# Order and buffers at the seam between attention and the gated layer of a fused fp32 kernel

## The chip, the cores and the metric

The kernel runs on one core of a Trainium2 chip. The metric is the device time of one execution in microseconds (us), median over the runs. The engines are named as in the profile: PE is TensorE (matmuls; PEld its weight loads), DVE is VectorE, ACT is ScalarE, POOL is GpSimd, SP is SyncE, whose queue issues the DMAs. The engines run side by side, each its own instructions in order, and meet through semaphores.

## The reference

Three stages follow each other, all in fp32. B = 4 batches, 8 heads, 1152 tokens that are pooled in twos to 576 queries, head size 64.

```python
def _attn_ref(q, k, v):
    q_pool = q.reshape(B, H, S // 2, 2, D).mean(axis=3)
    scores = (1 / sqrt(D)) * q_pool @ k.transpose(0, 1, 3, 2)
    attn = softmax(scores)                      # with 1e-9 in the sum
    return attn @ v                             # x: (4, 576, 512)

def _moe_ref(x, w_in, g_ln, w_sg, b_sg, w_out):
    h = gelu(x @ w_in)                          # tanh form, (4, 576, 1024)
    u, v = h[..., :512], h[..., 512:]
    v_n = (v - mean(v)) / sqrt(var(v) + 1e-6) * g_ln
    v_s = einsum('ts,bsd->btd', w_sg, v_n) + b_sg[None, :, None]
    return x + (u * v_s) @ w_out
```

A third stage (a token and a channel product with residuals) follows and isn't touched.

## The kernel before

**Attention.** The 32 heads go in 16 pairs (NP = 16; i is the pair). A pair has NS = 9 steps: steps 0 to 3 are query tiles of head 0, step 4 the remainder of both heads, steps 5 to 8 tiles of head 1. A step's work is a pipeline over the engines: PE makes the scores (L687, or L673 to L675 for step 4), DVE takes them out of PSUM with the row maximum (`take`, L1140), ACT makes the exponentials (`exps`, L950), DVE the reciprocal of the sum (`recip`, L1147 and L1149), POOL the normalisation (`norm`, L541), PE 18 transposes of it (`transpose_p`, L638), ACT and DVE copy these out to the tile pT (`evac_p`, L937 and L1155). The transposes of a step are made LAG = 4 steps after its scores. The value products of a pair (`values`, L704) are spread over the steps of the next pair by PV_STEPS: steps 0 to 3 hold head 0, steps 4 to 8 head 1. A finished head is copied from its PSUM bank to the tile xT by ACT and DVE together (`acc_copy`, L937 and L1160; semaphores acc_by_act and acc_by_dve).

After the last pair the same nine steps run once more without scores (`tail=True`, i = NP, L741, L983, L1184): this is the drain. Its steps 0 to 3 still transpose and evacuate steps 5 to 8 of the last pair, and hold the values of head 0; steps 4 to 8 hold only the values of head 1.

**Gated layer.** Products are made in fp32 out of three products of rounded parts: each operand is split in a high part (fp32r, a copy) and a low part (the difference). x of a batch is four slabs of 128 channels by 576 tokens: ACT copies to x_h (`x_hi_of`), DVE subtracts to x_l (`x_lo_of`, L1197). w_sg is split likewise in five rows (`sg_hi` on ACT, `sg_lo` on DVE, L1202). The weights are split by POOL (L501 the copy, L549 the subtraction), two units of them for w_out (wo) at the start of this layer.
PE makes in the order of the list GELU the value tiles v0 and v1 (`v_tile(b, m)`, 12 matmuls of 512 columns), then u0 (`pair(b, 0)`, 24 matmuls of 288), v2, v3, v4, u1, u2, u3. Each of them goes through the gelu: ACT `square`, DVE `poly` (L1209), ACT `tanh`, DVE `gelu` (L1226 for v, to the tile v_f). A v tile is then normalised: DVE statistics (L1229, L1230, L1232 to var_e), POOL the power (`norm_rstd`, L600), DVE `norm_v` (L1239), ACT n_h, DVE `norm_lo` (L1247). v_tile(b, 2) waits until gelu(b, 0) has freed its PSUM bank, v_tile(b, 3) for gelu(b, 1). DVE's order in batch 0 is gelu(0, 0), poly(0, 2), norm_v(0, 0), gelu(0, 1).

**The seam.** The tiles of the gated layer (context ctx2) lie over those of attention (ctx1) in the order in which both are declared. PE (L831, L832), ACT (L987), DVE (L1188), POOL (L591) and SP (L469) all wait there for acc_by_act and acc_by_dve to reach 2 * NP, that is, for the last copy of the last head. Then ACT copies the four x_h slabs, sg_hi(0), sg_hi(1), square(0, 0) and so on, DVE subtracts the x_l slabs, and PE starts v_tile(0, 0), which waits for x_split slab by slab. POOL starts its split of wo, and SP loads b_row, g_col and the weights of the third stage.

Of the kernel before, what the change touches and what calls it, by code (L numbers as in the profile page):

```python
# [27 lines left out]
PV_STEPS = ((0, range(0, 3)), (0, range(3, 5)), (0, range(5, 7)), (0, range(7, 9)),  # L28
            (1, range(0, 1)), (1, range(1, 3)), (1, range(3, 5)), (1, range(5, 7)), (1, range(7, 9)))
# [6 lines left out]
def at(i, per, off):  # L36

    return i * per + off
# [16 lines left out]
def build(nc, q, k, v, x_w_in, g_ln, w_sg, b_sg, w_out, w_tok1, w_tok2, w_ch1, w_ch2, out):  # L55
    NP, _, S = k.shape
    B, D = out.shape[0], v.shape[-1]
    H = 2 * NP // B
    SQ = S // 2
    DM = H * D  # L60
    KT_N = DM // P
    FF = x_w_in.shape[1]
    HF = FF // 2
# [4 lines left out]
    SPP = NP // B  # L68
# [3 lines left out]
    TT = QT_N  # L72
# [8 lines left out]
    def rows(t):  # L81
        return P if t < TT - 1 else QL
# [19 lines left out]
    def sb(ctx, name, shape, dt=F32):  # L102
        return ctx.enter_context(nc.sbuf_tensor(name, shape, dt))

    def sem(name):
        return top.enter_context(nc.semaphore(name))

    with top:
        ps = top.enter_context(nc.psum_tensor("ps", [P, 8, 512], F32))
        ident = sb(top, "ident", [P, P])  # L110
        xT = sb(top, "xT", [P, NP, SQ])
# [8 lines left out]
        ctx1 = ExitStack()  # L120
# [6 lines left out]
        ql2 = sb(ctx1, "ql2", [P, 2, QC], F32R)  # L127
        k_over = sb(ctx1, "k_over", [P, 2, 2, CK], F32R)
        q_over = sb(ctx1, "q_over", [P, 2, 4 * P], F32R)
        v_sb = sb(ctx1, "v_sb", [P, 2, KB, D])  # L130
        prob = sb(ctx1, "prob", [P, P_BUFS, S])
        ctx0 = ExitStack()
        k_two = sb(ctx0, "k_two", [P, S])
        q_two = sb(ctx0, "q_two", [P, 2, 4 * P])
# [10 lines left out]
        rsum = sb(ctx1, "rsum", [P, NS])  # L145
        ctx1.close()

        ctx2 = ExitStack()
        sg_h = sb(ctx2, "sg_h", [P, TT, SQ], F32R)
        sg_l = sb(ctx2, "sg_l", [P, TT, SQ], F32R)  # L150
        wo_h = sb(ctx2, "wo_h", [P, HF // P, DM], F32R)
        wo_l = sb(ctx2, "wo_l", [P, HF // P, DM], F32R)
        b_row = sb(ctx2, "b_row", [P, SQ])
        g_col = sb(ctx2, "g_col", [P, HF // P])
        x_h = sb(ctx2, "x_h", [P, KT_N, SQ], F32R)
        x_l = sb(ctx2, "x_l", [P, KT_N, SQ], F32R)
        n_h = sb(ctx2, "n_h", [P, TT, HF], F32R)
        n_l = sb(ctx2, "n_l", [P, TT - 1, HF], F32R)
        u_T = sb(ctx2, "u_T", [P, HF // P, SQ])
        gbuf = sb(ctx2, "gbuf", [P, 3, SQ])  # L160
        v_f = sb(ctx2, "v_f", [P, 3, HF])
        bst = sb(ctx2, "bst", [P, 3, 6])
        mv = sb(ctx2, "mv", [P, 3, 2])
        var_e = sb(ctx2, "var_e", [P, 3])
        rstd = sb(ctx2, "rstd", [P, 3])
        mixed = sb(ctx2, "mixed", [P, SQ])
        gate = sb(ctx2, "gate", [P, 2, SQ])
        ctx2b = ExitStack()
        sb(ctx2b, "behind_attention", [P, SG_PAD])
        sg_raw = sb(ctx2b, "sg_raw", [P, TT, SQ])  # L170
# [58 lines left out]
        s_taken = sem("s_taken")  # L229
# [8 lines left out]
        acc_by_act = sem("acc_by_act")  # L238
        acc_by_dve = sem("acc_by_dve")
# [3 lines left out]
        x_hi = sem("x_hi")  # L243
        x_split = sem("x_split")
# [372 lines left out]
        def _(pe):  # L617
# [120 lines left out]
                    step(i + 1, 0, s)  # L738
            for s in range(NS):
                step(NP - 1, 1, s)  # L740
            for s in range(NS):  # L741
                step(NP, 0, s, tail=True)

            def three(acc, wh, wl, xh, xl, start, stop):
# [14 lines left out]
            def v_tile(b, m):  # L759

                r = rows(m)
                if m == 4:
                    pe.wait_ge(res_done, at(b, 4, RES_N - 1))
                else:
                    pe.wait_ge(gelu_done, at(b, GT, GELU_N + (V_AT[m - 2] + 1 if m >= 2 else 0)))
                if m == 0 and not isinstance(b, int):
                    pe.wait_ge(mix_done, at(b, 4, -3))
                acc = ps[0:r, V_BANK[m], :]
                for kt in range(KT_N):
                    sl = slice(m * P, m * P + r)  # L770
                    if m == 0:
                        pe.wait_ge(x_split, at(b, KT_N, kt + 1))
                    ins = three(acc, x_h[:, kt, sl], x_l[:, kt, sl], wi_h[:, kt, HF:FF], wi_l[:, kt, HF:FF],
                                kt == 0, kt == KT_N - 1)
                ins.then_inc(v_mm, 1)
# [52 lines left out]
                    pair(b, 8 + f, [(wo_h[:, kt, sl], wo_l[:, kt, sl], g_h[:, kt, :], g_l[:, kt, :])  # L828
                                    for kt in range(HF // P)])

            pe.wait_ge(acc_by_act, 2 * NP)  # L831
            pe.wait_ge(acc_by_dve, 2 * NP)  # L832
            pe.wait_ge(w_split, U_WO)
            v_tile(0, 0)
            v_tile(0, 1)
            with pe.Fori(0, B - 1) as b:
                gated(b, False)
            gated(B - 1, True)
# [94 lines left out]
        def _(act):  # L933
            sc = nc.scalar

            def copy(o, i_):
                return sc.activation(o, i_, ACT.Copy)  # L937
# [27 lines left out]
            def step(i, s, first=False, tail=False):  # L965

                if s >= LAG and not tail:
                    evac_p(i, s - LAG)
                elif s < LAG and not first:
                    evac_p(i - 1, s - LAG + NS)  # L970
                if not first and s in (TAIL_STEP - 1, NS - 1):
                    acc_copy(i - 1, 0 if s == TAIL_STEP - 1 else 1)
                if s >= 1 and not tail:
                    exps(i, s - 1)
                elif s == 0 and not first:
                    exps(i - 1, NS - 1)
# [3 lines left out]
            with act.Fori(1, NP) as i:  # L980
                for s in range(NS):
                    step(i, s)
            for s in range(NS):  # L983
                step(NP, s, tail=True)


            act.wait_ge(acc_by_act, 2 * NP)  # L987
            act.wait_ge(acc_by_dve, 2 * NP)

            def slab(b):  # L990
                return xT[:, bass.ds(b * SPP, SPP), :]

            def x_hi_of(b):
                for f in range(KT_N):
                    copy(x_h[:, f, :], xT[:, b * SPP + f, :]).then_inc(x_hi, 1)

            def sg_hi(j):
                copy(sg_h[:, j, :], sg_raw[:, j, :]).then_inc(sgT_hi, 1)

            def square(b, e):  # L1000
                kind, n = GELU[e]
                if kind == "v":
                    act.wait_ge(v_mm, at(b, TT, n + 1))
                else:
                    act.wait_ge(pair_mm, at(b, 12, n + 1))
                act.wait_ge(gelu_done, at(b, GT, e + 1))
                h, buf = gelu_of(e)

                sc.activation(buf, h, ACT.Square, scale=(0.044715 * GC) ** 0.5).then_inc(squared, 1)
# [25 lines left out]
                    square(b + 1, 1)  # L1035
                    tanh(b + 1, 0)

            x_hi_of(0)
            act.wait_ge(sg_in, 32)
            sg_hi(0)  # L1040
            sg_hi(1)
            square(0, 0)
            sg_hi(2)
            square(0, 1)
            sg_hi(3)
            sg_hi(4)
            tanh(0, 0)
# [55 lines left out]
        def _(dve):  # L1103
            ve = nc.vector
# [52 lines left out]
            def acc_copy(i, a):  # L1157

                dve.wait_ge(acc_ready, at(i, 4, 2 * a + 2))
                ve.tensor_copy(xT[PH * a:PH * a + PH, i, HALF:SQ], ps[PH:P, ACC_BANK, 0:HALF]).then_inc(acc_by_dve, 1)  # L1160

            def step(i, s, first=False, tail=False):

                if s >= LAG and not tail:
                    evac_p(i, s - LAG)
                elif s < LAG and not first:
                    evac_p(i - 1, s - LAG + NS)
                if s >= 2 and not tail:
                    recip(i, s - 2)
                elif s < 2 and not first:  # L1170
                    recip(i - 1, s - 2 + NS)
                if not first and s in (TAIL_STEP - 1, NS - 1):
                    acc_copy(i - 1, 0 if s == TAIL_STEP - 1 else 1)
                if not tail:
                    take(i, s)
                    if first:
                        first_q(s)
# [3 lines left out]
            with dve.Fori(1, NP) as i:  # L1181
                for s in range(NS):
                    step(i, s)
            for s in range(NS):  # L1184
                step(NP, s, tail=True)


            dve.wait_ge(acc_by_act, 2 * NP)  # L1188
            dve.wait_ge(acc_by_dve, 2 * NP)

            def slab(b, f):
                return xT[:, b * SPP + f, :]

            def x_lo_of(b):
                for f in range(KT_N):
                    dve.wait_ge(x_hi, at(b, KT_N, f + 1))
                    ve.tensor_tensor(x_l[:, f, :], slab(b, f), x_h[:, f, :].bitcast(F32), ALU.subtract)\  # L1197
                        .then_inc(x_split, 1)

            def sg_lo(j):  # L1200
                dve.wait_ge(sgT_hi, j + 1)
                ve.tensor_tensor(sg_l[:, j, :], sg_raw[:, j, :], sg_h[:, j, :].bitcast(F32), ALU.subtract)\  # L1202
                    .then_inc(sgT_lo, 1)

            def poly(b, e):

                dve.wait_ge(squared, at(b, GT, e + 1))
                h, buf = gelu_of(e)
                ve.scalar_tensor_tensor(out=buf, in0=buf, scalar=GC, in1=h, op0=ALU.add, op1=ALU.mult)\  # L1209
                    .then_inc(z_ready, 1)  # L1210
# [86 lines left out]
                    ve.tensor_tensor(x_f, ps[:, b0:b0 + 2, 0:HALF], x_f, ALU.add).then_inc(res_done, 1)  # L1297

            head = Chain(dve, gelu_chain, 0)
            x_lo_of(0)  # L1300
            sg_lo(0)
            sg_lo(1)
            poly(0, 0)
            sg_lo(2)
            poly(0, 1)
            sg_lo(3)
            sg_lo(4)
            gelu(0, 0, head)
# [103 lines left out]
```

## Time and profile before

| | us |
|---|---|
| median of 3 runs | 1042.06 |
| lowest and highest run | 1040.93, 1042.2 |
| the profiled execution | 1043.86 |
| its span, first to last instruction | 1042.0 |
| busy in it: PE | 1004.9 |
| DVE | 590.4 |
| ACT | 452.6 |
| POOL | 381.7 |
| mean granted clock of PE, share of full | 0.988 |

All positions in the text are us from the start of the span. Busy shares are averages over stages with different limits; what one stage waits for is read from the timeline of that stage. Matmuls overlap in the pipeline, so a group's length is a little under the sum of its means. A page row and a row of a timeline merge neighbouring instructions of a kind: "8.09 ... x4" means four instructions in 8.09 us. The granted clock in a list of windows is 1.00 at 2.4 GHz and 0.50 at 1.2 GHz.

### The profile page before, as it was taken

Reading aid. Unit: us, or ns where it says so; the run is one execution under the profiler, and the core shown is the slowest. Engines: PE = TensorE matmul, PEld = TensorE weight load, DVE = VectorE, ACT = ScalarE, POOL = GpSimd, SP = SyncE. Lnnn points to the kernel's source line nnn. Section 1 sums busy time; section 2 is a strip of 40 time slices with the busy share of each in tenths; the row PEclk is TensorE's granted clock in tenths of the full one; section 3 lists DMA queues with packets and bytes.
Section 4 is the critical chain, followed back from the end, with each engine's and each line's share of the span. In section 5 each row is a group of like instructions: output and inputs, shape, how many; then the busy total and the mean of one; then the engine's idle time right before and its main releaser. Section 6 shows DMA issues by size and latency. Waiting matters only on the chain.

```text
span 1042.0 us, 23588 instructions
## 1 busy us (share of the span) xinstructions
PE 1004.9 (96%) x8948; PEld 824.1 (79%) x8948; DVE 590.4 (57%) x1167; ACT 452.6 (43%) x851; POOL 381.7 (37%) x296
## 2 busy tenths in 40 slices
PE   7899999999999998979999999999999999999998
PEld 7677777777777766659999998988888888888898
DVE  5787878777777776669495857445312113121121
ACT  3677777777777776635151514143111101111011
POOL 3877777777777786531010102278000000000000
PEclk9899999999999999989999999999999999999999
DMA  5644444444444433310000000133000101001010
GB/s 163 191 115 114 113 113 113 113 113 113 113 113 113 113 88 95 122 37 1 1 0 0 0 0 2 53 104 108 1 1 1 40 0 40 0 0 40 0 41 21
DMA packets 34017, 65.40 MB, mean 63 GB/s; under 512 B 6208, under 2 KB 14784, under 8 KB 33984
## 3 DMA queue, kind: packets, MB, share of 16 engines
q1 hardware_dynamic: 33824, 64.34, 21.6%
q10 hardware_dynamic: 160, 0.59, 0.2%
q8 instruction: 24, 0.39, 0.2%
q14 instruction: 9, 0.07, 0.0%
HBM read 42.93 MB, written 4.72 MB: 46 GB/s over the span
## 4 chain that ended last, share of the span: by engine, by line
PE 68%; issue 22%; DVE 5%; POOL 2%; DMA 1%; ACT 0%; DVEq 0%; SPq 0%; POOLq 0%; ACTq 0%
PE ps L704 13%; PE ps L746 12%; PE ps L747 12%; PE ps L748 12%; PE ps L687 10%; PE ps L638 6%; DVE prob L1140 2%; PE ps L673 1%; POOL rstd L600 1%; DVE pT L1155 1%; PE ps L675 1%; PE ps L674 1%; DMA q_two<-in_q 1%; DMA q_raw<-in_q 0%; POOL prob L541 0%
## 5 line engine op out<-in xcount | busy, mean ns | idle before, releaser
L1140 DVE TENSOR_SCALAR_CACHE_REDUCE prob<-ps 128x1152 f32<-128x1152 f32 x144 | 195.5, 1358 | 73.9 <-PE ps L687 55.4
L541 POOL TENSOR_SCALAR prob<-prob,rsum 128x1152 f32<-128x1152 f32 x144 | 176.8, 1228 | 115.8 <-DVE rsum L1149 115.4
L950 ACT ACTIVATE prob<-prob,nmax 128x1152 f32<-128x1152 f32 x144 | 181.1, 1258 | 17.1 <-DVE prob L1140 10.3
L704 PE MATMUL ps<-pT,v_sb 128*64 128x288 f32 x1152 | 173.1, 423 | 2.5 <-DVE xT L1160 0.6
L1360 DVE SCALAR_TENSOR_TENSOR f_l<-ps,f_h 128x512 fp32r<-128x512 f32 (+1 forms) x60 | 38.3, 638 | 222.7 <-ACT f_h L1090 222.7
L937 ACT ACTIVATE pT<-ps 128x512 f32<-128x512 f32 (+1 forms) x288 | 109.5, 432 | 100.0 <-PE ps L638 99.9
L1090 ACT ACTIVATE f_h<-ps 128x512 fp32r<-128x512 f32 (+1 forms) x60 | 33.3, 555 | 256.4 <-PE ps L748 256.4
L687 PE MATMUL ps<-k_over,q_over 64*128 64x288 f32 x744 | 132.7, 311 | 4.0 <-DVE prob L1140 4.0
L687 PEld LDWEIGHTS ps<-k_over,q_over 64*128 64x128 f32 x744 | 103.7, 187 | 24.2 <-DVE prob L1140 22.7
L638 PEld LDWEIGHTS ps<-ident,prob 64*128 64x128 f32 x2592 | 100.3, 140 | 20.8 <-issue 20.7
L638 PE MATMUL ps<-ident,prob 64*128 64x64 f32 x2592 | 107.7, 225 | 6.6 <-POOL prob L541 3.6
L704 PEld LDWEIGHTS ps<-pT,v_sb 128*64 128x64 f32 x1152 | 72.1, 137 | 44.8 <-issue 9.0
L1155 DVE COPY pT<-ps 128x512 f32<-128x512 f32 x144 | 98.9, 687 | 12.7 <-PE ps L638 12.7
L747 PE MATMUL ps<-u_l,c_h 128*128 128x512 f32 (+1 forms) x240 | 88.3, 368 | 0.0
L746 PE MATMUL ps<-u_h,c_h 128*128 128x512 f32 (+1 forms) x240 | 88.3, 368 | 0.0
L748 PE MATMUL ps<-u_h,c_l 128*128 128x512 f32 (+1 forms) x240 | 88.3, 368 | 0.0
L746 PE MATMUL ps<-f_h,c_h 128*128 128x512 f32 (+1 forms) x240 | 88.3, 368 | 0.0
L747 PE MATMUL ps<-f_l,c_h 128*128 128x512 f32 (+1 forms) x240 | 88.3, 368 | 0.0
L748 PE MATMUL ps<-f_h,c_l 128*128 128x512 f32 (+1 forms) x240 | 88.3, 368 | 0.0
L687 PE MATMUL ps<-kh,qh 64*128 64x288 f32 x248 | 85.9, 346 | 0.0
L600 POOL TENSOR_TENSOR rstd<-var_e,minus_half 128x1 f32<-128x1 f32 (+1 forms) x20 | 15.5, 775 | 174.9 <-DVE var_e L1232 174.9
L687 PE MATMUL ps<-kl,qh 64*128 64x288 f32 x248 | 72.9, 294 | 0.0
(141 smaller groups left out, 2175.6 us busy)
## 6 DMA issues: line engine op xcount, KB each, us to landing
q_raw<-in_q SPq DMA_DIRECT2D x16, 640.0 KB, 5.0
k_raw<-in_k SPq DMA_DIRECT2D x16, 576.0 KB, 4.0
v_sb<-in_v SPq DMA_DIRECT2D x32, 288.0 KB, 2.8
k_over<-kh SPq DMA_DIRECT2D x31, 144.0 KB, 2.5
k_over<-kl SPq DMA_DIRECT2D x31, 144.0 KB, 2.6
out_x<-xT SPq DMA_DIRECT2D x4, 1024.0 KB, 4.2
q_over<-qh SPq DMA_DIRECT2D x31, 128.0 KB, 2.3
q_over<-ql SPq DMA_DIRECT2D x31, 128.0 KB, 2.4
```

The costliest lines, as they stand in the source:

```text
L541: g.tensor_scalar(sl, sl, rsum[:, s:s + 1], 0.0, ALU.mult, ALU.add).then_inc(norm_done, 1)
L638: ins = te.transpose(dst, prob[half, PROB_BUF[s], j * P:(j + 1) * P], ident[half, half])
L687: ins = te.matmul(ps[:, 2 * m + t, 0:CK], w, x, start=(term == 0), stop=(term == 2))
L704: ins = te.matmul(ps[PH * c:PH * c + PH, ACC_BANK, 0:n], v_sb[:, a, j, :], pT[:, a, j, c * n:c * n + n], start=(j == 0), stop=(j == KB - 1))
L746: te.matmul(acc, wh, xh, start=start, stop=False)
L747: te.matmul(acc, wh, xl, start=False, stop=False)
L748: return te.matmul(acc, wl, xh, start=False, stop=stop)
L937: return sc.activation(o, i_, ACT.Copy)
L950: sc.activation(sl, sl, ACT.Exp, scale=-1.0, bias=nmax[:, s:s + 1], accum_out=esum[:, s:s + 1]).then_inc(exp_done, 1)
L1140: ve.tensor_scalar(prob[:, PROB_BUF[s], :].rearrange("p (c n) -> p c n", c=SCORE_BANKS), ps[:, 0:SCORE_BANKS, 0:CK], -SCALE, BIG, ALU.mult ...
L1155: ve.tensor_copy(pT_of(s, 1), trans(1)).then_inc(pT_by_dve, 1)
L1360: ve.scalar_tensor_tensor(out=f_l[:, f % F_N, 0:n], in0=ps[:, f % F_N, 0:n], scalar=0.0, in1=f_h[:, f % F_N, 0:n].bitcast(F32), op0=ALU.ma ...
```

## The change

The tiles of ctx2 are declared in another order: x_h, x_l, sg_h, sg_l first, which puts them where k, q and their splits were; then gbuf, v_f, the small ones, n_h, gate, mixed; wo_h, wo_l, n_l, u_T, b_row, g_col come last of them. In ctx1, prob and v_sb exchange places. The waits of PE, ACT and DVE for the last copy of the accumulator are gone at this place; those of POOL and SP stay. ACT and DVE run only steps 0 to 3 of the drain, with the splits of x of batch 0 between them, and copy head 1's result later, behind square(0, 1) on ACT and behind poly(0, 1) on DVE. PE runs steps 0 to 3 of the drain, then v_tile(0, 0) and v_tile(0, 1), then the values of head 1.

```diff
-        v_sb = sb(ctx1, "v_sb", [P, 2, KB, D])
         prob = sb(ctx1, "prob", [P, P_BUFS, S])
+        v_sb = sb(ctx1, "v_sb", [P, 2, KB, D])
...
         ctx2 = ExitStack()
+        x_h = sb(ctx2, "x_h", [P, KT_N, SQ], F32R)
+        x_l = sb(ctx2, "x_l", [P, KT_N, SQ], F32R)
         sg_h = sb(ctx2, "sg_h", [P, TT, SQ], F32R)
         sg_l = sb(ctx2, "sg_l", [P, TT, SQ], F32R)
...
             for s in range(NS):
                 step(NP - 1, 1, s)
-            for s in range(NS):
+            for s in range(TAIL_STEP):
                 step(NP, 0, s, tail=True)
...
-            pe.wait_ge(acc_by_act, 2 * NP)
-            pe.wait_ge(acc_by_dve, 2 * NP)
+            pe.wait_ge(s_taken, NP * NS)
             pe.wait_ge(w_split, U_WO)
             v_tile(0, 0)
             v_tile(0, 1)
+            for s in range(TAIL_STEP, NS):
+                values(NP - 1, *PV_STEPS[s])
...
-            act.wait_ge(acc_by_act, 2 * NP)
-            act.wait_ge(acc_by_dve, 2 * NP)
...
-            x_hi_of(0)
+            step(NP, 0, tail=True)
+            x_hi_tile(0, 0)
+            step(NP, 1, tail=True)
+            x_hi_tile(0, 1)
+            step(NP, 2, tail=True)
+            x_hi_tile(0, 2)
+            x_hi_tile(0, 3)
+            step(NP, 3, tail=True)
             act.wait_ge(sg_in, 32)
             sg_hi(0)
             sg_hi(1)
             square(0, 0)
             sg_hi(2)
             square(0, 1)
+            acc_copy(NP - 1, 1)
             sg_hi(3)
             sg_hi(4)
             tanh(0, 0)
...
-            dve.wait_ge(acc_by_act, 2 * NP)
-            dve.wait_ge(acc_by_dve, 2 * NP)
...
-            x_lo_of(0)
+            step(NP, 0, tail=True)
+            step(NP, 1, tail=True)
+            x_lo_tile(0, 0)
+            step(NP, 2, tail=True)
+            x_lo_tile(0, 1)
+            x_lo_tile(0, 2)
+            step(NP, 3, tail=True)
+            x_lo_tile(0, 3)
             sg_lo(0)
             sg_lo(1)
             poly(0, 0)
             sg_lo(2)
             poly(0, 1)
+            acc_copy(NP - 1, 1)
             sg_lo(3)
             sg_lo(4)
             gelu(0, 0, head)
```

`x_hi_tile(b, f)` and `x_lo_tile(b, f)` are the bodies of the loops of `x_hi_of` and `x_lo_of`, one slab each.

## Rows read from the trace of the kernel before

**Rows 1.** The page, part 1: busy time, share of the span, instructions.
```profile
PE 1004.9 (96%) x8948; PEld 824.1 (79%) x8948; DVE 590.4 (57%) x1167; ACT 452.6 (43%) x851; POOL 381.7 (37%) x296
```

**Rows 2.** Windows, PE: window, length, PE busy, granted clock, DMA share, GB/s.
```profile
411.20:413.50 2.30, 0.21 (x4) 1.00 0.04 16
413.50:420.30 6.80, 5.87 (x56) 0.50 0.16 47
...
451.04:461.20 10.16, 7.24 (x16) 0.50 0.23 66
```

**Rows 3.** Timeline, PE: start, length, line, operation, count, [idle before <-releaser].
```profile
438.49 0.77 PE L638 MATMUL ps<-ident,prob 64*128 64x64 f32 x18
...
442.97 4.59 PE L704 MATMUL ps<-pT,v_sb 128*64 128x288 f32 x36 [0.64 <-DVE xT L1160]
450.01 0.47 PE L746 MATMUL ps<-wi_h,x_h 128*128 128x512 f32 x1 [2.45 <-DVE x_l L1197]
...
452.76 0.79 PE L746 MATMUL ps<-wi_h,x_h 128*128 128x512 f32 x1 [1.83 <-DVE x_l L1197]
...
462.58 0.30 PE L746 MATMUL ps<-x_h,wi_h 128*128 128x288 f32 x1
...
466.09 0.50 PE L746 MATMUL ps<-wi_h,x_h 128*128 128x512 f32 x1
...
469.09 0.50 PE L746 MATMUL ps<-wi_h,x_h 128*128 128x512 f32 x1
```

**Rows 4.** Timeline, DVE, at the seam and in the first gelus of batch 0.
```profile
438.27 0.16 DVE L1149 RECIPROCAL rsum<-lsum 128x1 f32<-128x1 f32 x1
...
447.60 0.46 DVE L1160 COPY xT<-ps 64x288 f32<-64x288 f32 x1 [4.73 <-PE ps L704]
448.97 8.09 DVE L1197 TENSOR_TENSOR x_l<-xT,x_h 128x576 fp32r<-128x576 f32 x4 [0.91 <-ACT x_h L937]
...
448.97 0.89 DVE L1197 TENSOR_TENSOR x_l<-xT,x_h 128x576 fp32r<-128x576 f32 x1 [0.91 <-ACT x_h L937]
...
452.63 4.43 DVE L1197 TENSOR_TENSOR x_l<-xT,x_h 128x576 fp32r<-128x576 f32 x2
...
467.89 0.54 DVE L1239 TENSOR_SCALAR v_f<-v_f,mv,rstd 128x512 f32<-128x512 f32 x1
468.35 0.68 DVE L1226 SCALAR_TENSOR_TENSOR v_f<-gbuf,ps 128x512 f32<-128x512 f32 x1
```

**Rows 5.** Timeline, POOL: the last normalisation, the first split of wo, the first rstd.
```profile
438.60 1.23 POOL L541 TENSOR_SCALAR prob<-prob,rsum 128x1152 f32<-128x1152 f32 x1 [0.54 <-DVE rsum L1149]
448.21 1.04 POOL L501 TENSOR_SCALAR wo_h<-stage 128x1024 fp32r<-128x1024 f32 x1 [8.39 <-DVE xT L1160]
449.34 2.75 POOL L549 TENSOR_TENSOR wo_l<-stage,wo_h 128x1024 fp32r<-128x1024 f32 x1
...
467.25 0.56 POOL L600 TENSOR_TENSOR rstd<-var_e,minus_half 128x1 f32<-128x1 f32 x1 [10.80 <-DVE var_e L1232]
```

**Rows 6.** Groups up to 520 us: line, engine, operation, count, busy, mean ns, idle before.
```profile
L549 POOL TENSOR_TENSOR wi_l<-stage,wi_h 128x1024 fp32r<-128x1024 f32 x4 | 9.5, 2379 | 0.0
...
L1202 DVE TENSOR_TENSOR sg_l<-sg_raw,sg_h 128x576 fp32r<-128x576 f32 x5 | 3.6, 749 | 0.0
```

**Rows 7.** Timeline, ACT: the evacuation of step 6, the four x_h copies.
```profile
437.48 0.77 ACT L937 ACTIVATE pT<-ps 128x512 f32<-128x512 f32 x2
...
448.15 2.40 ACT L937 ACTIVATE x_h<-xT 128x576 fp32r<-128x576 f32 x4 [0.15 <-DVE xT L1160]
```

**Rows 8.** DMA issues, 425 to 475 us: count, KB each, us to landing.
```profile
sg_raw<-in_moe_w_sg SPq DMA_DIRECT2D x1, 288.0 KB, 6.8
...
g_col<-in_moe_g_ln SPq DMA_DIRECT2D x1, 2.0 KB, 3.1
```

**Rows 9.** Timeline in batch 3: POOL's subtraction and DVE's polynomial beside it.
```profile
649.15 2.71 POOL L549 TENSOR_TENSOR t_l<-stage,t_h 128x1024 fp32r<-128x1024 f32 x1
...
649.63 0.75 DVE L1209 SCALAR_TENSOR_TENSOR gbuf<-gbuf,ps 128x576 f32<-128x576 f32 x1
```

More of the change, by code:

```diff
@@ L129, in build @@
         q_over = sb(ctx1, "q_over", [P, 2, 4 * P], F32R)
+        prob = sb(ctx1, "prob", [P, P_BUFS, S])
         v_sb = sb(ctx1, "v_sb", [P, 2, KB, D])
-        prob = sb(ctx1, "prob", [P, P_BUFS, S])
         ctx0 = ExitStack()
@@ L148, in build @@
         ctx2 = ExitStack()
+        x_h = sb(ctx2, "x_h", [P, KT_N, SQ], F32R)
+        x_l = sb(ctx2, "x_l", [P, KT_N, SQ], F32R)
         sg_h = sb(ctx2, "sg_h", [P, TT, SQ], F32R)
         sg_l = sb(ctx2, "sg_l", [P, TT, SQ], F32R)
[L151 to L159, printed above, removed]
         gbuf = sb(ctx2, "gbuf", [P, 3, SQ])
@@ L165, in build @@
         rstd = sb(ctx2, "rstd", [P, 3])
+        n_h = sb(ctx2, "n_h", [P, TT, HF], F32R)
+        gate = sb(ctx2, "gate", [P, 2, SQ])
         mixed = sb(ctx2, "mixed", [P, SQ])
-        gate = sb(ctx2, "gate", [P, 2, SQ])
+        wo_h = sb(ctx2, "wo_h", [P, HF // P, DM], F32R)
+        wo_l = sb(ctx2, "wo_l", [P, HF // P, DM], F32R)
+        n_l = sb(ctx2, "n_l", [P, TT - 1, HF], F32R)
+        u_T = sb(ctx2, "u_T", [P, HF // P, SQ])
+        b_row = sb(ctx2, "b_row", [P, SQ])
+        g_col = sb(ctx2, "g_col", [P, HF // P])
         ctx2b = ExitStack()
@@ L982, in _, with x_hi_tile @@
                     step(i, s)
-            for s in range(NS):
-                step(NP, s, tail=True)
-            act.wait_ge(acc_by_act, 2 * NP)
-            act.wait_ge(acc_by_dve, 2 * NP)
             def slab(b):
                 return xT[:, bass.ds(b * SPP, SPP), :]
+            def x_hi_tile(b, f):
+                copy(x_h[:, f, :], xT[:, b * SPP + f, :]).then_inc(x_hi, 1)
             def x_hi_of(b):
                 for f in range(KT_N):
-                    copy(x_h[:, f, :], xT[:, b * SPP + f, :]).then_inc(x_hi, 1)
+                    x_hi_tile(b, f)
             def sg_hi(j):
@@ L1183, in _, with x_lo_tile @@
                     step(i, s)
-            for s in range(NS):
-                step(NP, s, tail=True)
-            dve.wait_ge(acc_by_act, 2 * NP)
-            dve.wait_ge(acc_by_dve, 2 * NP)
             def slab(b, f):
                 return xT[:, b * SPP + f, :]
+            def x_lo_tile(b, f):
+                dve.wait_ge(x_hi, at(b, KT_N, f + 1))
+                ve.tensor_tensor(x_l[:, f, :], slab(b, f), x_h[:, f, :].bitcast(F32), ALU.subtract)\
+                    .then_inc(x_split, 1)
             def x_lo_of(b):
                 for f in range(KT_N):
-                    dve.wait_ge(x_hi, at(b, KT_N, f + 1))
-                    ve.tensor_tensor(x_l[:, f, :], slab(b, f), x_h[:, f, :].bitcast(F32), ALU.subtract)\
-                        .then_inc(x_split, 1)
+                    x_lo_tile(b, f)
             def sg_lo(j):
```

## Prediction

> **What bounds the kernel now.** I read the page first: TensorE is busy for 1004.9 of 1042.0 us [rows 1], so time is to be had only where it waits or runs at the lower of its two clocks. The granted clock in five-microsecond windows is at 1.2 GHz in only four places; two lie near the seam between attention and the first gated layer, at 413.5 to 420.3 and at 451.04 to 461.2 us [rows 2]. Then I read the timeline of each engine across the seam. TensorE ends the value products of head 1 of the last pair at 442.97 + 4.59 = 447.56 us, starts the first value tile of batch 0 at 450.01, its second input slab only at 452.76, the first pair of batch 0 at 462.58, and the fourth value tile, v_tile(0,3), at 469.09 [rows 3]. From there to the end of the batch no TensorE wait longer than 0.4 us follows. So 442.97 to 469.09, 26.1 us, is the stretch that the change acts on. Its work at 2.4 GHz would be: head 1's values 4.6 us, three value tiles of 2.9 (466.09 to 469.09 with a small gap), and 24 matmuls of the pair at 0.133 = 3.2, in all 16.5. The other 9.6 us are waiting and half clock.
>
> Why it waits there: VectorE's four x_l subtractions take 8.09 us instead of 4 x 0.75. The first ends at 448.97 + 0.89 = 449.86, the second at about 452.7 [rows 4]. GpSimd runs its wo copies and subtractions at just that time; they end at 449.25 and 452.09 [rows 5]. A VectorE subtraction with both inputs in SBUF thus ends 0.6 us after the GpSimd instruction that was running when it started, and GpSimd's own subtraction grows from 2.38 [rows 6] to 2.75 us, having waited for the first VectorE one. That is a lock between the two, not a slow instruction: alone, the same shape takes 0.749 [rows 6].
>
> **The change, part by part.** The layout itself costs nothing and moves no wait: x_h, x_l and sg now lie over k, q, kh, kl, qh, ql and the over copies, whose last readers are the scores of step 8, ended before 434.4. It lets the splits start before head 1's values are read. No instruction is added or removed, and the prob and v_sb exchange changes no buffer's use.
>
> *The drain.* x_hi(0) of batch 0 (one ScalarE copy, 2.40 / 4 = 0.60) goes ahead of the evacuation of step 6, which ScalarE starts at 437.48 [rows 7]. It can start at about 437.3, so that evacuation starts at 437.95 and ends at 438.7; TensorE's next transposes, at 438.49 [rows 3], go to 438.8: **+0.3 us**. x_hi(1) lies in ScalarE's idle time before the next evacuation (1.08 us, by the timeline). x_lo(0) starts on VectorE after the reciprocal of 438.27 [rows 4], about 438.4, just ahead of GpSimd's last normalisation at 438.60 [rows 5]. First there, it takes 0.75, and the normalisation ends near 440.3 instead of 439.83, still ahead of the transposes that wait for it (440.44 before, about 440.75 now). If the order falls the other way, x_lo(0) ends at 440.4 and delays an evacuation by 0.7. Bounds 0 to +1.0, taken +0.3, because each engine has an idle stretch of about that size there. x_lo(1) and (2) delay VectorE's last evacuation to about 441.85, which only head 1's values need. TensorE ends head 0's values at 442.6, against 442.3 before, and the 0.64 us before head 1 (waiting for the accumulator's copy) is covered by the value tiles. x_lo(3) runs from 443.1 to 443.85, and TensorE wants it after nine matmuls, at 444.7: hidden. The weights wi were split by 431.7, and sg_raw was issued at 433 and landed 6.8 us later [rows 8], before its first use near 443.6.
>
> *TensorE's order.* Two value tiles 442.6 to 448.45 (2 x 2.92), head 1's values to 453.05, pair(0,0) to 456.25. Before, that point was 465.8. So far **9.6 us** are saved, and all of the waiting in the stretch is gone.
>
> *What comes late next.* GpSimd's four wo instructions, SP's b_row, g_col and tok loads still wait for the last copy of the accumulator, now the one at about 453.15 to 453.6 (0.46 [rows 4]). So GpSimd starts 0.15 later, 453.75, as it did 448.21 against 448.06. Behind head 1's accumulator copy on ScalarE stand sg_hi(3), sg_hi(4), tanh(0,0); on VectorE sg_lo(3), sg_lo(4), gelu(0,0), and v_tile(0,2) waits for that gelu. sg_lo(3) starts at 454.2 and is locked out until the first wo copy ends (453.75 + 1.04 = 454.8), so it ends at 455.4. wo_l follows from 455.35 to 457.6, sg_lo(4) is held to 458.2, gelu(0,0) runs to 458.85 and v_tile(0,2) starts at 458.9, **2.6 us after pair(0,0) ended**. It ends at 461.8.
> GpSimd's second wo pair runs 457.55 to 459.1 and 459.2 to 461.55, and it is in order: rstd(0,0), ready for it at about 460, starts only at 461.6 and ends 0.56 later [rows 5]. From there I copy the distances of before: norm_v starts 0.64 after rstd's start, gelu(0,1) 0.46 after norm_v, v_tile(0,3) 0.74 after that gelu (467.25, 467.89, 468.35, 469.09 [rows 3, 4, 5]). That gives 463.5. A second wait of TensorE, 1.7 us. Without either, v_tile(0,3) would start near 459.2. b_row and g_col are issued by 454.1 and land 3.1 us later [rows 8], behind VectorE's gelu(0,0) but ahead of its wait for them at 460: no cost.
> **469.09 - 463.5 = 5.6 us saved** at the fourth value tile, at full clock.
> One SBUF input and one in PSUM, as gelu has, is not locked out: a polynomial step at 649.63 takes 0.75 inside a GpSimd subtraction of 2.71 [rows 9]. If gelu(0,0) were locked out after all, it would end at 459.7, v_tile(0,2) at 462.6, still ahead of 463.5.
> The Trainium skill says the same of the lock (SBUF — State Buffer, "The single rule"): whichever of the two starts first holds the shared port for its whole instruction, and a VectorE instruction with at most one SBUF input outside the two-port modes is free. It speaks against this change, since it makes the moved GpSimd work land on sg_lo. With the port shared evenly instead, the two sg_lo would take about twice 0.75 each and the first wait would be about 1 us, but the queue behind rstd would stay.
>
> *The clock.* After 3 us of waiting, the clock fell at 413.5 and stayed at 1.2 GHz for 6.8 us with 5.87 us of work in it, so it cost 2.9. The other stretch was 10.2 us with 7.24 of work, 3.6 [rows 2]. In the new seam TensorE works for 2.9 us between two waits of 2.6 and 1.7, much like 450.01 to 452.76 now. So I expect one low stretch of 6.8 us. If it begins at 461.3, it runs 4.6 us past 463.5 and costs 2.3; if it begins after 463.5, 3.4. I take **+2.8**. Bounds: nothing, and 5.1 (10.2 us all on work). The low stretch of before costs nothing extra, since it lies in the 26.1 us already.
>
> Sum: -5.6 + 2.8 = -2.8 us. The profiled execution took 1043.86 us (span 1042.0 and 1.9 around it), 1.8 above the median 1042.06; it would go to 1041.1, and the median to **1039.3**.
>
> **Rivals.** (a) *The clock holds.* Each wait is shorter than the 3.0 of 411.4 and there is work between. Against: the fall at 451.04 came after a wait of 2.45 and one of 1.83 with 0.9 of work between. Gives 1042.06 - 5.6 = 1036.5. Chance 0.15.
> (b) *The clock stays low for long*, 10.2 us as at 451.04, or from v_tile(0,2) on. From 461.3 to 471.5 it costs 4.0, fully on work 5.1; 1040.5 to 1041.6, taken 1041.0. For: two waits in close order gave the long stretch of before. Chance 0.20.
> (c) *The lock costs sg_lo nothing* (GpSimd is done or late). Then gelu(0,0) ends at 456.1 and the first wait is gone, but rstd waits behind 6.84 us of GpSimd work, v_tile(0,3) starts at 462.7, saved 6.4, clock 2.8: 1038.4. Chance 0.08.
> (d) *Slower: two low stretches in a row on a TensorE that no longer waits.* Before, about 3 us of the low time was waiting and free; now nearly all of it would be work. The place is 458.9 to 476, the price half of the low time after 463.5. From 11.2 us of it the saving is gone. 6.8 and 10.2 together are 17 us, 8.5 us of cost: 1045.0. Against: no low stretch in this trace exceeds 10.2 us, and work from 463.5 on is unbroken. Chance 0.07.
> That the tiles don't run ahead of head 1 at all is excluded: every semaphore they wait for is reached by 443.9.
>
> **How the numbers follow.** The forecast's case has 0.50, (a) 0.15, (b) 0.20, (c) 0.08, (d) 0.07. About 0.2%, 2.1 us, is what a measurement of this kernel can tell from no change, so faster means below 1040.0 and slower above 1044.1. The forecast's case spans 1038.8 to 1039.9, and as the three runs spread over 1.3 us, 0.40 of its 0.50 counts as faster. With (a) and most of (c): faster 0.62. Same: 0.10 of the forecast, (b), and a rest: 0.31. Slower 0.07. The range goes from under (a), with 0.7 for a drain cheaper than counted, to past (b): 1035.8 to 1042.0; outside lie (d) and the far ends.
>
> **What would show it.** Right: the first value tile at about 442.6 and head 1's values at 448.5; sg_lo(4) at about 2.9 us; TensorE idle for 2 to 3 us ahead of v_tile(0,2), released by v_f, and for 1 to 2 ahead of v_tile(0,3), with rstd starting as wo_l ends; v_tile(0,3) at 463 to 464; one low stretch of 6.8 us from about 461. Wrong: no wait before v_tile(0,2) (the lock term), a fourth tile at 460 (the GpSimd queue), full clock throughout, or a drain that ends over 1 us later.

## The result

| | before | after |
|---|---|---|
| median, us | 1041.8 (5 runs) | 1035.95 (5 runs) |
| lowest and highest run | 1040.93, 1042.2 | 1034.82, 1036.04 |
| the profiled execution, and its span | 1043.86, 1042.0 | 1035.03, 1033.2 |

The ratio of the runs is 0.994, with an interval from 0.9927 to 0.9952: 5.85 us less. Forecast were 1039.3 us, a gain of 2.8, and a range of 1035.8 to 1042.0. The direction was right, the gain was twice the forecast, and the time sits at the very edge of the range.

The page of the changed kernel, span and part 1, against [rows 1]:

```profile
span 1033.2 us, 23586 instructions
...
PE 1000.4 (97%) x8948; PEld 822.5 (80%) x8948; DVE 587.7 (57%) x1167; ACT 452.4 (44%) x851; POOL 382.3 (37%) x296
```

TensorE's busy time fell by 4.5 us with the same 8948 matmuls, so half clock has gone too. The lines of its code have moved by one (L747 to L749 are the three products, L705 the values). Its timeline at the seam, with the same columns as [rows 3]:

```profile
434.83 0.77 PE L639 MATMUL ps<-ident,prob 64*128 64x64 f32 x18 [0.15 <-ACT pT L941]
...
438.57 0.50 PE L747 MATMUL ps<-wi_h,x_h 128*128 128x512 f32 x1
...
444.24 4.59 PE L705 MATMUL ps<-pT,v_sb 128*64 128x288 f32 x36
448.75 0.40 PE L747 MATMUL ps<-x_h,wi_h 128*128 128x288 f32 x1
...
454.78 0.50 PE L747 MATMUL ps<-wi_h,x_h 128*128 128x512 f32 x1 [2.58 <-DVE v_f L1231]
...
459.25 0.40 PE L747 MATMUL ps<-wi_h,x_h 128*128 128x512 f32 x1
```

The three waits for x_l are gone, and head 1's values have no wait ahead. What is left is one wait of 2.58 us, ahead of v_tile(0,2), for gelu(0,0). VectorE and GpSimd at that place (as [rows 4] and [rows 5]):

```profile
434.46 0.74 DVE L1198 TENSOR_TENSOR x_l<-xT,x_h 128x576 fp32r<-128x576 f32 x1
...
450.04 3.96 DVE L1207 TENSOR_TENSOR sg_l<-sg_raw,sg_h 128x576 fp32r<-128x576 f32 x2 [0.69 <-ACT sg_h L941]
454.03 0.69 DVE L1231 SCALAR_TENSOR_TENSOR v_f<-gbuf,ps 128x512 f32<-128x512 f32 x1
...
457.92 0.55 DVE L1244 TENSOR_SCALAR v_f<-v_f,mv,rstd 128x512 f32<-128x512 f32 x1 [1.25 <-POOL rstd L601]
458.38 0.68 DVE L1231 SCALAR_TENSOR_TENSOR v_f<-gbuf,ps 128x512 f32<-128x512 f32 x1
```

```profile
434.71 1.58 POOL L542 TENSOR_SCALAR prob<-prob,rsum 128x1152 f32<-128x1152 f32 x1 [0.53 <-DVE rsum L1158]
449.51 1.06 POOL L502 TENSOR_SCALAR wo_h<-stage 128x1024 fp32r<-128x1024 f32 x1 [13.21 <-DVE xT L1169]
450.65 2.74 POOL L550 TENSOR_TENSOR wo_l<-stage,wo_h 128x1024 fp32r<-128x1024 f32 x1
453.36 1.55 POOL L502 TENSOR_SCALAR wo_h<-stage 128x1024 fp32r<-128x1024 f32 x1
454.99 2.37 POOL L550 TENSOR_TENSOR wo_l<-stage,wo_h 128x1024 fp32r<-128x1024 f32 x1
457.33 0.56 POOL L601 TENSOR_TENSOR rstd<-var_e,minus_half 128x1 f32<-128x1 f32 x1
```

The lock has moved from x_l to sg_lo(3) and sg_lo(4), 3.96 us for the two, and rstd(0,0) starts in the very moment when the last wo_l ends. GpSimd's last normalisation takes 1.58 us instead of 1.23, beside x_lo(0), which had started 0.25 us ahead of it.

**One clock for all traces.** The two spans differ by 8.8 us, the medians by 5.85. To see why, I take all positions from the start of VectorE's last take of scores, before and after:

```profile
434.44 1.36 DVE L1140 TENSOR_SCALAR_CACHE_REDUCE prob<-ps 128x1152 f32<-128x1152 f32 x1
```

```profile
430.56 1.36 DVE L1149 TENSOR_SCALAR_CACHE_REDUCE prob<-ps 128x1152 f32<-128x1152 f32 x1
```

Ahead of that point the change touches only the places of prob and v_sb, yet it comes 3.9 us earlier. The eighth take from the last is at 408.82 and 408.42 us, so 3.5 of the 3.9 us arise behind it. The cause is the hole at 411 us, in which TensorE stands idle: GpSimd stands in its queue behind a late weight load and TensorE behind GpSimd. The waits between 395 and 425 us (who waited for whom, total, times, longest) are, before and after:

```profile
POOL wi_h L501 <- DMA stage<-in_moe_w_in: 4.4, 1, 4.4
PE ps L638 <- POOL prob L541: 3.0, 1, 3.0
```

```profile
POOL wi_h L502 <- DMA stage<-in_moe_w_in: 3.1, 1, 3.1
PE ps L639 <- POOL prob L542: 1.8, 1, 1.8
```

In the first profile before, the clock fell there as well [rows 2]; in the first profile after, it didn't. Further profiles of both kernels (below) put the last take at 431.6 for the kernel before and at 434.2 for the changed one: these 3.9 us are a matter of the execution, and no part of the change.

The working of the prediction, position by position, all from the last take, in us:

| event | forecast | first profile after | second profile after |
|---|---|---|---|
| first value tile starts | 8.2 | 8.0 | 7.9 |
| pair(0,0) starts | 18.6 | 18.2 | 18.1 |
| v_tile(0,2) starts | 24.5 | 24.2 | 24.1 |
| v_tile(0,3) starts | 29.1 | 28.7 | 28.5 |

The kernel before reached v_tile(0,3) 34.65 us after its last take in the first profile (469.09 - 434.44), and 34.1 in a second.

### The profile page after: what moved, and what is told of

Same layout as the page of the kernel before. It is cut to its first block, busy times and chain, and to the rows that moved or that the text cites. A ratio compares the mean times of both kernels' runs of the same rounds, so it can differ in the third digit from the quotient of the medians.

```text
span 1033.2 us, 23586 instructions
## 1 busy us (share of the span) xinstructions
PE 1000.4 (97%) x8948; PEld 822.5 (80%) x8948; DVE 587.7 (57%) x1167; ACT 452.4 (44%) x851; POOL 382.3 (37%) x296
## 4 chain that ended last, share of the span: by engine, by line
PE 69%; issue 21%; DVE 5%; POOL 3%; DMA 1%; ACT 1%; DVEq 0%; SPq 0%; POOLq 0%; ACTq 0%
PE ps L705 12%; PE ps L747 12%; PE ps L749 12%; PE ps L748 12%; PE ps L688 10%; PE ps L639 6%; DVE prob L1149 2%; PE ps L674 1%; POOL rstd L601 1%; DVE pT L1164 1%; PE ps L676 1%; PE ps L675 1%; DMA q_two<-in_q 1%; DMA q_raw<-in_q 1%; POOL prob L542 0%
## 5 line engine op out<-in xcount | busy, mean ns | idle before, releaser
L705 PE MATMUL ps<-pT,v_sb 128*64 128x288 f32 x1152 | 171.0, 419 | 1.9
L688 PEld LDWEIGHTS ps<-k_over,q_over 64*128 64x128 f32 x744 | 102.9, 186 | 24.2 <-DVE prob L1149 22.7
L705 PEld LDWEIGHTS ps<-pT,v_sb 128*64 128x64 f32 x1152 | 71.1, 136 | 43.8 <-issue 8.2
L747 PE MATMUL ps<-u_h,c_h 128*128 128x512 f32 (+1 forms) x240 | 88.3, 368 | 0.0
L749 PE MATMUL ps<-u_h,c_l 128*128 128x512 f32 (+1 forms) x240 | 88.3, 368 | 0.0
L747 PE MATMUL ps<-f_h,c_h 128*128 128x512 f32 (+1 forms) x240 | 88.3, 368 | 0.0
L749 PE MATMUL ps<-f_h,c_l 128*128 128x512 f32 (+1 forms) x240 | 88.3, 368 | 0.0
L688 PE MATMUL ps<-kh,ql 64*128 64x288 f32 x248 | 72.6, 293 | 0.0
```

The costliest lines, as they stand in the source:

```text
L688: ins = te.matmul(ps[:, 2 * m + t, 0:CK], w, x, start=(term == 0), stop=(term == 2))
L705: ins = te.matmul(ps[PH * c:PH * c + PH, ACC_BANK, 0:n], v_sb[:, a, j, :], pT[:, a, j, c * n:c * n + n], start=(j == 0), stop=(j == KB - 1))
L747: te.matmul(acc, wh, xh, start=start, stop=False)
L749: return te.matmul(acc, wl, xh, start=False, stop=stop)
```

## The experiments

The theory ahead of the runs was this: the seam is now set by GpSimd's split of wo, by the lock and by the queue ahead of rstd; the order of tiles and heads matters only through what it does to those two; and the low clock cost nothing here because it fell on time in which TensorE would have waited. Rivals: the order of the tiles is the gain in itself; only the lock counts; the clock's low price was luck.

### e1_wo_late

```diff
             pool.wait_ge(acc_by_act, 2 * NP)
             pool.wait_ge(acc_by_dve, 2 * NP)
-            for u in range(U_WO, U_T1):
-                split_w(u)
...
+            for m in range(5):
+                norm_rstd(0, m)
+            for u in range(U_WO, U_T1):
+                split_w(u)
+            for m in range(5, TT):
+                norm_rstd(0, m)
-            with pool.Fori(0, B) as b:
+            with pool.Fori(1, B) as b:
```

> The changed kernel with GpSimd's split of wo moved behind the five rstd of batch 0. Theory: what is left at the seam of the changed kernel is GpSimd's work, by its lock on the two sg_lo (3.96 us instead of 1.5) and by its queue ahead of rstd(0,0). Without it v_tile(0,2) follows pair(0,0) at 452.1 and v_tile(0,3) starts at 455.3 instead of 459.25, so 3.9 us less: 1032.0 us. Rival: the lock only moves, to norm_lo and x_lo of batch 1 some 20 us later, and costs TensorE as much there: 1035 to 1036 us.

Measured: 1033.67 us, ratio to the kernel before 0.9934 (0.9913 to 0.9954). v_tile(0,3) starts 24.7 us after the last take, 4.0 earlier than in the changed kernel; the wait ahead of v_tile(0,2) is gone. But the lock came back at the place that the rival named: the last norm_lo of batch 0 stands beside the split, and the first mixing product waits for it:

```profile
473.83 2.08 DVE L1255 TENSOR_TENSOR n_h<-v_f,n_h 64x512 fp32r<-64x512 f32 x1
...
475.96 0.40 PE L756 MATMUL ps<-sg_h,n_h 128*128 128x288 f32 x1 [2.02 <-DVE n_h L1255]
```

So half of the 4.0 us is given back 19 us later. The theory was right in the place and the size of the first part, the rival was right that the lock moves; the forecast of 1032.0 us was too low by that wait.

### e2_before_wo_late

The same move of wo in the kernel before, nothing else.

> The kernel before with the same move of the split of wo, order and layout of before. Theory: in the kernel before the larger loss is GpSimd's lock on x_l (8.09 us for four). Without it x_l takes 3 us, the first slab still comes 2.45 us after head 1, the other waits of 1.83 and 1.20 us and most of the half clock go, pair(0,0) starts near 456 instead of 462.6: 6 to 7 us less, 1035 to 1036 us, as much as the change itself. Rival: the wait for the accumulator and the order of the tiles are the loss; then this gives at most 2 us (1040).

Measured: 1037.62 us, ratio 0.9971 (0.9948 to 0.9993). VectorE's four x_l subtractions, TensorE's wait for them, and a window behind it (its start and end, length, busy time, granted clock, DMA share, GB/s):

```profile
446.31 2.77 DVE L1200 TENSOR_TENSOR x_l<-xT,x_h 128x576 fp32r<-128x576 f32 x4 [0.91 <-ACT x_h L940]
...
447.22 0.47 PE L749 MATMUL ps<-wi_h,x_h 128*128 128x512 f32 x1 [2.32 <-DVE x_l L1200]
```

```profile
448.00:451.40 3.40, 3.40 (x10) 0.52 0.12 18
```

The subtractions take 2.77 us, against 8.09 for the same line before [rows 4]. v_tile(0,3) starts 29.2 us after the last take instead of 34.65, and a wait of 1.50 us for norm_lo follows as in e1. The split of wo, in its old place, was thus the cause of more than half of what the seam cost: moving it alone brings v_tile(0,3) to within 0.5 us of where the whole change puts it (28.7), with TensorE's order and the late x split left as they were. By the medians it gains 3.7 us (1041.34 to 1037.62, the runs of before being those taken beside e2), and the whole change 5.85. The forecast of 1035 to 1036 was 2 us too low: pair(0,0) starts 22.6 us after the last take where the forecast had 21.6, as half clock still falls on the first value tiles, and the 1.50 us come on top.

The change has a worth beside the split of wo, too. With wo late in both, v_tile(0,3) starts 4.5 us earlier in the changed kernel than in the kernel before (e1 24.7, e2 29.2), and the medians differ by 4.0. e2 still has the wait of 2.32 us for x_l and 1.6 us of half clock behind it (its 24 matmuls of v_tile(0,0) and v_tile(0,1) take 6.97 us, in e1 5.37); in e1, where x is split in the drain, neither is there.

### e3_heads_first and e4_heads_first_copy_early

e3 swaps the two blocks on TensorE; the splits of x stay in the drain.

```diff
+            for s in range(TAIL_STEP, NS):
+                values(NP - 1, *PV_STEPS[s])
             v_tile(0, 0)
             v_tile(0, 1)
-            for s in range(TAIL_STEP, NS):
-                values(NP - 1, *PV_STEPS[s])
```

> The changed kernel, but TensorE makes the values of head 1 before the first two value tiles; the splits of x stay in the drain. Theory: the order between the heads buys little, as TensorE's work is the same: 0.35 us for the accumulator's copy ahead of head 1, and the copy of head 1 comes 1.2 us later behind poly(0,1), so GpSimd is later by that: 1 to 1.5 us slower than the changed kernel, 1037.2 us. Rival: the tiles between the heads are what hides the wait for x; then it is 2.5 us or more slower, above 1038.4.

e4 has this and, on both engines, the copy of head 1 ahead of the first gelu:

```diff
             sg_hi(0)
             sg_hi(1)
+            acc_copy(NP - 1, 1)
             square(0, 0)
             sg_hi(2)
             square(0, 1)
-            acc_copy(NP - 1, 1)
```

> As e3_heads_first, with the copies of head 1 on ScalarE and VectorE ahead of square(0,0) and poly(0,0) instead of behind square(0,1) and poly(0,1). Theory: e3 was 4 us slower than the changed kernel because its late copy started GpSimd's split late, and the order of tiles and heads itself matters little. GpSimd then starts 14.1 us after the last scores are taken out (21.2 in e3, 18.95 in the changed kernel), is done before rstd(0,0) is ready, and v_tile(0,3) starts at 27 against 28.7 after that point: 1.7 us less than the changed kernel, 1034.3 us. Rival: the tiles between the heads are themselves the gain; then it stays at e3's 1039.9.

Measured: e3 1039.91 us, ratio 0.9994 (0.9977 to 1.0012), all of the gain gone; e4 1034.28 us, ratio 0.9936 (0.9915 to 0.9956), at least as fast as the changed kernel. By its number alone e3 looked like its rival, but its trace has no wait for x at all. TensorE's waits and GpSimd's split in e3:

```profile
455.43 0.50 PE L747 MATMUL ps<-wi_h,x_h 128*128 128x512 f32 x1 [1.76 <-DVE v_f L1231]
462.11 0.80 PE L747 MATMUL ps<-wi_h,x_h 128*128 128x512 f32 x1 [3.67 <-DVE v_f L1231]
...
452.50 1.55 POOL L502 TENSOR_SCALAR wo_h<-stage 128x1024 fp32r<-128x1024 f32 x1 [15.49 <-DVE xT L1169]
...
460.31 0.56 POOL L601 TENSOR_TENSOR rstd<-var_e,minus_half 128x1 f32<-128x1 f32 x1
```

The copy of head 1 stands behind poly(0,1) and so behind two tiles that now come 5.5 us later. GpSimd starts 21.2 us after the last take instead of 18.95, and rstd(0,0) follows the split. v_tile(0,3) starts 30.8 us after the last take, 2.2 later than in the changed kernel. The 3.67 us of waiting are followed by a low stretch of 6.8 us, 6.0 of it on work (0.80 us for a matmul of 0.50), which costs 2.5 us more up to pair 8 of the batch, the first product with w_out. The forecast, 1037.2, had counted 1.2 us for the later GpSimd and no low clock. In e4 the copy is early and GpSimd with it:

```profile
445.38 1.05 POOL L502 TENSOR_SCALAR wo_h<-stage 128x1024 fp32r<-128x1024 f32 x1 [8.44 <-DVE xT L1169]
...
455.90 0.56 POOL L601 TENSOR_TENSOR rstd<-var_e,minus_half 128x1 f32<-128x1 f32 x1 [3.10 <-DVE var_e L1237]
```

rstd now waits for VectorE, not the other way round, and v_tile(0,3) starts at 26.6 us. With x split in the drain, e4's first value tile starts 13.5 us after the last take, right behind head 1; in e2, with the same order on TensorE and the late split, at 15.4. So the tiles between the heads are not the gain, and the early split is a part of it. What counts in this order is when the last copy of the accumulator lets GpSimd go.

### e5_layout_only and e10_small_last

e5 is the kernel before with only the two blocks of declarations of the change.

> The kernel before with the changed kernel's layout alone. Theory: within 0.1% of the kernel before, 1041.8 us, with the same 8 us of x_l. Rival: where the tiles lie costs or gains by itself; then it moves by over 1 us.

Measured: 1042.57 us, ratio 1.0015 (0.9995 to 1.0036), no difference that can be told from noise, and the four x_l take 8.08 us. One thing differed in its trace: from pair 8 of a batch to pair 8 of the next it takes 54.30 us, where the kernel before takes 54.50 and e2, with the old layout, 54.48. e10 is the kernel before with this alone:

```diff
-        b_row = sb(ctx2, "b_row", [P, SQ])
-        g_col = sb(ctx2, "g_col", [P, HF // P])
         x_h = sb(ctx2, "x_h", [P, KT_N, SQ], F32R)
...
         gate = sb(ctx2, "gate", [P, 2, SQ])
+        b_row = sb(ctx2, "b_row", [P, SQ])
+        g_col = sb(ctx2, "g_col", [P, HF // P])
```

> The kernel before with b_row and g_col (4 words per partition) declared behind the other tiles of the gated layer, so that x, n, u and the rest no longer lie behind a tile of 16 bytes. Theory: the 0.18 us per batch that the layout alone gained (54.49 to 54.30 us from pair 8 to pair 8 of the next batch) comes from where a tile starts; then the period is 54.3 here too. Rival: it comes from the order of the large tiles; then 54.5.

The tiles moved are b_row, 576 words per partition, and g_col, 4 words; the expectation's "4 words" is true of g_col alone. Measured, in one run of 1043.06 us: a period of 54.24 us. One form of matmul from 500 to 640 us, its mean in ns before and in e10:

```profile
L748 PE MATMUL ps<-wi_h,x_l 128*128 128x512 f32 x48 | 18.9, 394 | 0.0
```

```profile
L748 PE MATMUL ps<-wi_h,x_l 128*128 128x512 f32 x45 | 17.6, 391 | 0.0
```

So 0.2 us per batch hang on where tiles start, and the order of the large tiles isn't needed for it. Which of the two moved tiles matters, and why, isn't shown. It is a part of the change's gain that the prediction put at nothing: the changed kernel's three periods (54.31, 54.31, 49.13) are 0.46 us shorter than those before (54.50, 54.50, 49.21). The medians of e5 don't show it, as it is smaller than their spread.

### e6_gelu_first

```diff
             square(0, 1)
-            acc_copy(NP - 1, 1)
             sg_hi(3)
             sg_hi(4)
             tanh(0, 0)
+            acc_copy(NP - 1, 1)
```

and the same on VectorE around sg_lo(3), sg_lo(4) and gelu(0,0).

> The changed kernel with sg_hi, sg_lo(3), sg_lo(4), tanh and gelu(0,0) ahead of the copy of head 1, so that GpSimd's lock finds no subtraction while its queue stays ahead of rstd(0,0). Theory: v_tile(0,2) follows pair(0,0) without a wait, but v_tile(0,3) still waits for rstd: one wait of about 3.3 us in place of 2.6 and none. v_tile(0,3) starts 0.9 us earlier, but the low clock now falls on work behind it: 0 to 2.5 us slower than the changed kernel, 1036 to 1038.4 us. Rival: only the lock counts, and it gains the 2.6 us: 1033.4 us.

Measured: 1036.81 us, ratio 0.9969 (0.9952 to 0.9987), inside the forecast. One of its ten runs took 1592.3 us at a mean granted clock of 0.557; the ratio leaves it out, and its cause is open. TensorE, and windows around its wait (window, length, busy, granted clock):

```profile
459.39 0.50 PE L747 MATMUL ps<-wi_h,x_h 128*128 128x512 f32 x1 [3.32 <-DVE v_f L1231]
```

```profile
456.10:459.39 3.29, 0.00 (x0) 1.00 0.58 190
...
460.80:464.20 3.40, 3.40 (x10) 0.53 0.00 0
464.20:467.00 2.80, 2.80 (x15) 1.00 0.00 0
```

The lock has nothing to hit, the two sg_lo take 1.42 us, and yet nothing is gained: the wait is 3.32 us for rstd alone, and the low clock, now at 460.8, lies wholly on work. From v_tile(0,3) to pair 8 it takes 37.1 us here (496.47 - 459.39) and 35.8 in e7 (491.90 - 456.13), where the clock doesn't fall, so 3.4 us of low clock cost 1.3. The first matmul of pair 8 in e6, and the two places in e7:

```profile
496.47 0.30 PE L747 MATMUL ps<-g_h,wo_h 128*128 128x288 f32 x1
```

```profile
456.13 0.50 PE L751 MATMUL ps<-wi_h,x_h 128*128 128x512 f32 x1
...
491.90 0.30 PE L751 MATMUL ps<-g_h,wo_h 128*128 128x288 f32 x1
```

"Only the lock counts" is refuted.

### e7_gelu_first_wo_later

e6, with GpSimd's order of e1 and a later start of the split. Against e1's order the only new line on GpSimd is:

```diff
             for m in range(5):
                 norm_rstd(0, m)
+            pool.wait_ge(pair_mm, 5)
             for u in range(U_WO, U_T1):
                 split_w(u)
```

> e6_gelu_first with GpSimd's split of wo behind the fifth pair of batch 0. Theory: no wait of TensorE over 0.4 us from the drain to pair 8; in e1_wo_late one of 2.02 us was left ahead of the first mixing product, where the split's lock fell on norm_lo(0,4). So 2.0 to 2.3 us less than e1's 1033.7: 1031.5 us. Rival: the split now locks out the gates and g_lo, and TensorE waits there as long ahead of pair 8: 1033.7 us.

Measured: 1032.54 us, ratio 0.9929 (0.9903 to 0.9955), the fastest of all. TensorE has no wait over 0.3 us from the first value tile to pair 8 of batch 0, which starts 60.25 us after the last take (64.3 in the changed kernel, 62.4 in e1, 70.4 before). The x_l of batch 1 are locked in turn, 6.68 us for the four against 2.76 in the changed kernel, and TensorE doesn't wait for them. Against e1 the trace shows the 2.2 us that were forecast; the medians, of runs taken at different times, differ by 1.1, and the 1031.5 us of the forecast were 1.0 too low.

### e8_before_again and e9_after_again

The two kernels unchanged, for second profiles.

> The kernel before, once more, for a second profile. Theory: of the 8.8 us between the spans of the two first profiles, 3.9 lie ahead of the seam and are the luck of one execution (a weight load that landed late at 412 us and a fall of the clock). From the last scores taken out to the end it takes 607.6 us if the clock is low for 10 us at the seam as in the first profile, and 605.5 to 606.5 if for 3.4. Rival: those 3.9 us belong to the kernel; then its last scores are taken out near 434.4 again, against 430.6 to 432.4 in the other kernels.

> The changed kernel once more. Theory: v_tile(0,3) starts 28.7 us after the last scores are taken out, as in its first profile, whatever the clock does, because a low stretch there falls on v_tile(0,2), behind which TensorE would wait for GpSimd's queue anyway; median within 1 us of 1036. Rival: the small cost of the clock in the first profile was luck, and here v_tile(0,3) or pair 8 of batch 0 comes 1 to 3 us later (pair 8 was 64.3 us after that point).

Measured: e8 1041.6 us, ratio 1.0011 (0.9993 to 1.003); v_tile(0,3) starts 34.1 us after the last take:

```profile
465.66 0.50 PE L746 MATMUL ps<-wi_h,x_h 128*128 128x512 f32 x1
```

The last take is at 431.6, 607.0 us from there to the end, with a low stretch of 10.2 us at the seam again, near the 607.6 expected for that. With the last take three microseconds earlier than in the first profile, the rival that the 3.9 us belong to the kernel falls. e9 1034.46 us, ratio 0.9947 (0.9914 to 0.9981), which is 1.5 below the 1036 of the forecast where 1 had been allowed; last take at 434.2, though its kernel is the changed one. Windows of e9 (first the wait, then v_tile(0,2), the second wait, what follows):

```profile
455.80:458.36 2.56, 0.00 (x0) 1.00 0.11 13
458.36:461.40 3.04, 3.04 (x12) 1.00 0.47 166
461.40:462.73 1.33, 0.00 (x1) 1.00 0.30 98
462.73:469.50 6.77, 6.77 (x33) 1.00 0.00 0
```

and the same stretch of the first profile after:

```profile
452.20:455.78 3.58, 1.00 (x4) 0.98 0.20 46
455.78:459.19 3.41, 3.41 (x9) 0.52 0.43 144
459.19:466.00 6.81, 6.81 (x35) 1.00 0.00 0
```

With the fall, v_tile(0,2) takes 4.4 us and v_tile(0,3) follows at once. Without it, it takes 3.0 us and TensorE waits for the 1.33 us left. v_tile(0,3) starts at 28.7 and 28.5 us: the low clock cost 0.2 us. Pair 8 starts at 64.3 us in both. Why the clock fell in one of the two executions and not in the other is open.

## Why the prediction was right in its path and wrong in its size

- **What bounds the seam.** Right: waiting and half clock around x_l, caused by GpSimd's lock. e2 shows it by moving GpSimd's split away and leaving all else: 5.45 of the 9.6 us go. The rest stood mostly in the wait for the first x_l and the half clock behind it.
- **The drain.** Forecast +0.3; the transposes of step 7 came 4.27 us after the last take instead of 4.05, +0.2. x_lo(0) came first and the normalisation grew, as told.
- **TensorE's order.** Head 1's values and pair(0,0) came 0.3 and 0.4 us earlier than forecast. Of this 0.15 us lie ahead of the first value tile; the value tiles' 24 matmuls, spaced by 0.228 us instead of 0.233, give 0.12: the layout, which I had put at nothing.
- **What comes late next.** Right: the lock on the two sg_lo (3.96 measured, 4.0 worked out), TensorE's wait of 2.6 us, rstd behind wo_l, the second wait (1.7 forecast, 1.33 in e9; covered by the low clock in the first profile). Gain at v_tile(0,3): forecast 5.6 us, measured 6.0 between the first profiles and 5.6 between the second ones.
- **The clock, the step that failed: the term was mis-sized.** Forecast +2.8, from two cases of 2.3 and 3.4; measured 0.2 in the first profile, and nothing in the second, where the clock didn't fall. The step took a low stretch of 6.8 us that began at 461.3 or later in before's time. It was 3.4 us long, and began at 459.7 in that time, so it lay inside v_tile(0,2). That tile was followed by a wait, as the prediction had worked out itself in its part on what comes late, without using it for the clock: whatever the clock takes from work ahead of a wait, the wait gives back. The price of 1.3 us for 3.4 us on work, as e6 shows, was the right kind of price, at the wrong place. The length was luck as far as the runs show: nothing here tells why it was 3.4 and not 6.8. As an estimate, 6.8 us from the same start would have put 3.4 on the unbroken work behind v_tile(0,3), and cost about the 1.3 us of e6.
- **The baseline.** I read the length of a low stretch from one execution, 6.8 and 10.2 us. Over the further traces 3.4 us is the most common. At the seam with the order of before it was 10.2 us in three traces (the first, e8, e10) and 3.4 in e5.
- **Rivals.** (a), the clock holds, is what e9 did, and its 1036.5 is 0.6 from the median. Its chance of 0.15 was too small, since for the time it needed no held clock, only a fall at a harmless place. (c) named the queue behind rstd as the second bound, which e6 shows. (b) and (d) did not occur.
- **The rest.** 5.6 to 6.0 us at the seam and about 0.5 of the layout make 6.1 to 6.5, against 5.85 of the medians. From the last take to the end the traces give 607.6 to 602.6 us between the first profiles, and 606.9 to 601.1 between the second. In the first profile after, one more fall of the clock at 657 us, behind a wait of 1.58, cost 1.5 us; it came in five of the twelve traces.

## What to carry to other kernels

When work moves past a wait, ask what the wait released on the idle engine: here GpSimd's weight split, let go by the last copy, locked VectorE and stood ahead of a tiny rstd. Moving that split by a few lines, in the kernel before, gained 3.7 us by the medians, where the whole change gained 5.85, or 7.0 when run again (e9); on top of the change it brought pair 8 of batch 0 another 1.9 us forward (e1), and the early split of x kept a worth of its own beside it (e1 against e2). Price a low-clock stretch only by the part of it that lies on work with no wait behind it. And compare traces from the last event that the change can't touch, since here 4 us of two profiles lay ahead of it.

## What the runs showed of the hardware

The same matmuls run 0.3 to 0.5% faster or slower with the place of their operands: 54.24 to 54.31 us per batch against 54.48 to 54.50 (e5, e10). In e10 it was enough to move b_row and g_col, 580 words per partition together, from ahead of the operands to behind them. Which of the two it is, and which operand, was not tried. A VectorE subtraction of two SBUF tiles ended 0.6 us after GpSimd's running instruction, beside a copy (449.86 against 449.25) as beside a subtraction (454.0 against 453.4, in the changed kernel), while gelu, with one input in PSUM, started at 454.03 beside GpSimd's second copy (453.36 + 1.55) and took its usual 0.69.
